# One program for the bias stage and attention, transposes ahead of scores, three more attention steps ahead of the MLP

## The chip, the core and the metric

The kernel runs on one core of a Trainium2 chip. The metric is the device time of one execution in microseconds. A core has TensorE (PE in the rows; its weight loads are PEld), VectorE (DVE), ScalarE (ACT), GpSimd (POOL) and SyncE (SP), which here only issues DMA transfers. Each engine runs its own list of instructions in order and waits on semaphores for the others.

## What is computed

Attention over 4 batches of 8 heads, 576 positions, 64 values a head, with a bias that a small network makes out of the distance of two positions; then two MLPs over the 2304 rows of 512 values.

```python
rel = (pos[:, None] - pos[None, :])
psi_rel, psi_i = log1p(abs(rel)), log1p(maximum(pos[:, None], 1.0))
x = (psi_rel / psi_i)[..., None]
bias = maximum(x @ w1 + b1, 0.0) @ w2              # 32 hidden values, 8 heads
scores = scale * q @ k.T + bias
attn = exp(scores - max) / (sum + 1e-9)
x = (attn @ v).transpose(0, 2, 1, 3).reshape(2304, 512)
h = x @ w_in;   x = (s * relu(h) ** 2 + b) @ w_out
h = x @ w2_in;  return (h - tanh(h)) @ w2_out      # d_ff is 2048 in both
```

## The kernel before

Every float32 operand of a large product is split in a rounded high part and a low part, so that a product is made of two or three matmuls. The program has three stretches.

**The bias stage.** 36 packs of 16 rows i. For each pack ScalarE and VectorE make two hidden tiles each (`hidden` and `maximum`), TensorE multiplies them by `w2_s` into one of four pairs of PSUM banks (`ps_f`, `ps_s`, `ps_t`, `ps_o`, in turn), ScalarE evicts the columns ahead of the diagonal and VectorE the mirrored ones behind it into `stage`, and SyncE stores the pack to the DRAM tensor `bias_flat`. A skewed view of it gives the bias rows of a head; `sp_bias` loads those of tile t into `bias_t`, which has one buffer for each tile. The hidden tiles have `HIDS` buffers, `stage` has four. This stage is a program block of its own, with a barrier of all engines at its end.

**Attention alone.** A head n is done in steps (n, t), t from 0 to 4, one for each tile of 128 query rows. A step carries three heads' work: scores of head n (`ps_s`, one pair of banks), VectorE's reduce L544, which adds the bias and takes the maximum, and ScalarE's exponential; transposes of head n-1's tile (L477, into `ps_t` and `ps_f` in turn while `alone`), ScalarE's rounding of it (`pth`, L490) and VectorE's low part (`ptl`, L556); and the value product of head n-1's previous tile (L442 and L444, `ps_o`). Step (n, 0) also ends head n-2: ScalarE copies the lower half (`o_tmp`), VectorE adds the halves into `x_raw`. The denominators are inverted on VectorE, transposed, stored in DRAM (`inv_rows`) and loaded again as a row for every partition (`inv_b`); in odd steps (n, 0) GpSimd scales two heads of `x_raw` by it (`pool_scale`). GpSimd also rounds k and makes the low parts of k, q and v of the heads to come; q and k have one raw buffer, so `load_qk` of head n+2 waits for the low parts of head n+1. The first 46 steps (`FIRST`) are done in this way.

**Mixed and MLP.** Then the MLP runs in units of 464 rows, 64 blocks of 12 matmuls each; after the blocks in `PLACES` of the first three units one attention step is put. `act_weights` and `pool_weights` split the weights three blocks ahead, `act_split` and `dve_split` split x.

```python
bias_t = tile("bias_t", [P, NT, S])
need(pe, min_done, n * NT + t)          # scores of a step wait for the reduce before
need(pe, pt_lo_done, v * NT + t - alone)
sp.wait_ge(min_done, n * NT + t + 1)    # SyncE, step (n, t), then bias rows of head n+1
```

Of the kernel before, what the change touches and what calls it, by code (L numbers as in the profile page):

```python
# [10 lines left out]
P = 128  # L11
# [7 lines left out]
HIDS = 3  # L19
VEC = 2  # L20
LATE = 2
RING = 4
# [4 lines left out]
def build(nc, qt, kt, vt, net, w2s, w2t, psi, lam, sb, w1, w2, w3, w4, out):  # L27
# [7 lines left out]
    HID = w2t.shape[0]  # L35
    G = P // HID
# [18 lines left out]
    FIRST = (H + 1) * NT + 1  # L55
# [5 lines left out]
    def step_at(u, k):  # L61

        if u >= B - 1 or k not in PLACES:
            return None
        return STEPS_AT[FIRST + u * H * NT + PLACES.index(k)]

# [12 lines left out]
    with ExitStack() as ctx:  # L79
# [26 lines left out]
        const_done = sem("const_done")  # L106
        hid_dve = sem("hid_dve")
        hid_act = sem("hid_act")
        no_const = sem("no_const")
# [94 lines left out]
        with ExitStack() as bctx:  # L204
            bb = lambda name, shape, dt=F32: bctx.enter_context(nc.sbuf_tensor(name, shape, dt))
            psi_t = bb("psi_t", [P, S])
            lam_c = bb("lam_c", [P, STEPS])
            inv_lam = bb("inv_lam", [P, STEPS])
            slope = bb("slope", [P, STEPS])
            net_c = bb("net_c", [P, 2])  # L210
            w1_c, b1_c = net_c[:, 0:1], net_c[:, 1:2]
            nb1_c = bb("nb1_c", [P, 1])
            w2_s = bb("w2_s", [P, G * H])
            w2_t = bb("w2_t", [HID, P])
            const = bb("const", [P, 1])
            hid = bb("hid", [P, HIDS, PACK, S])
            stage = bb("stage", [P, RES_BUFS, S + ROW])
            res = [ps_f, ps_s, ps_t, ps_o]

            def forward(pack):  # L220

                return S - pack * ROW

            def backward(pack):

                return pack * ROW + ROW - 1

            def reach(pack):

                n = max(forward(pack), backward(pack) + 1)  # L230
                return n + n % 2

            def chunks(pack):

                n = reach(pack)
                half = n // 2 + (n // 2) % 2
                parts = [(0, n)] if n <= BANK else [(0, half), (half, n)]
                return [(res[pack % RES_BUFS][:, c, 0:hi - lo], lo, hi) for c, (lo, hi) in enumerate(parts)]

            block = bctx.enter_context(nc.Block())  # L240

            def load_bias(sp, t):
                packs = min(PACKS, (t + 1) * P // ROW)
                for i in range(RES_BUFS):
                    sp.wait_ge(stage_stored[i], packs // RES_BUFS * DMA)
# [620 lines left out]
```

## Time and profile before

| | |
|---|---|
| three runs | 1181.2, 1181.64 and 1181.9 us, median 1181.64 |
| profiled execution | 1182.0 us, span of the trace 1180.2 us |
| TensorE busy | 1123.6 us, 95% of the span |
| ScalarE, VectorE, GpSimd busy | 720.2, 629.5 and 597.8 us |
| first bias hidden operation | 6.08 us |
| last mirrored bias row, start and length | 71.31 and 0.94 us |
| first attention reduce | 77.40 us |
| first MLP matmul | 180.49 us |
| DMA | 172.47 MB, most of it on SyncE's queue |

Times are counted from the start of the span. The engines' busy shares are means over stretches of very different kinds.

### The profile page before, as it was taken

The numbers are of one execution on the slowest core, as the hardware profiler recorded it, in microseconds if no ns is written. First come the engines' busy times: TensorE is split into PE (matmuls) and PEld (weight loads), VectorE is DVE, ScalarE is ACT, GpSimd is POOL, SyncE is SP. The second block draws the span as 40 slices with busy tenths as digits, with TensorE's granted clock in tenths as the row PEclk, the third lists the DMA queues.
The fourth block names the chain that finished last, engine by engine and source line by source line (L and its number), as shares of the span: only waits on it lengthen the run. The fifth ranks groups of instructions, "written<-read, shape, count | busy, mean of one in ns | idle before, by whom it ended". The sixth has DMA issues, their size and how long they took to land.

```text
span 1180.2 us, 17800 instructions
## 1 busy us (share of the span) xinstructions
PE 1123.6 (95%) x6306; PEld 995.0 (84%) x6306; DVE 629.5 (53%) x1090; ACT 720.2 (61%) x1362; POOL 597.8 (51%) x505
## 2 busy tenths in 40 slices
PE   4659878999999999999999999999999999999998
PEld 1138767999999999999999999999988888999998
DVE  5857775744675366447654754566344063260440
ACT  8957785755676477557665765676455264473552
POOL 1014545566465545655655555555455455555553
PEclk9879998999999999999999999999999999999999
DMA  3577773455445544554455454453233333433332
GB/s 127 209 249 200 217 211 93 151 172 178 139 155 159 175 152 142 163 157 141 162 167 171 138 160 156 149 162 125 81 115 107 107 101 105 131 109 124 97 111 75
DMA packets 69657, 172.47 MB, mean 146 GB/s; under 512 B 8704, under 2 KB 15680, under 8 KB 69568
## 3 DMA queue, kind: packets, MB, share of 16 engines
q1 hardware_dynamic: 69280, 171.24, 46.3%
q8 instruction: 51, 0.84, 0.3%
q14 instruction: 38, 0.31, 0.1%
q10 hardware_dynamic: 288, 0.07, 0.0%
HBM read 155.59 MB, written 15.69 MB: 145 GB/s over the span
## 4 chain that ended last, share of the span: by engine, by line
PE 85%; ACT 1%; issue 0%; DVE 0%; ACTq 0%
PE ps_f L652 23%; PE ps_f L654 23%; PE ps_f L653 23%; PE ps_t L477 6%; PE ps_o L442 3%; PE ps_o L444 3%; PE ps_s L464 3%; PE ps_s L465 3%; PE ps_s L458 0%; ACT p_t L499 0%; ACT pth L490 0%; DVE ptl L556 0%; ACT wh L602 0%; DVE xl L628 0%; DVE p_t L544 0%
## 5 line engine op out<-in xcount | busy, mean ns | idle before, releaser
L609 POOL TENSOR_TENSOR wl<-w_raw,wh 128x512 fp32r<-128x512 f32 x320 | 418.3, 1313 | 441.5 <-ACT wh L602 441.3
L652 PE MATMUL ps_f<-xh,wh 128*128 128x464 f32 (+1 forms) x640 | 239.4, 374 | 5.0 <-issue 5.0
L652 PE MATMUL ps_f<-gh,wh 128*128 128x464 f32 (+1 forms) x640 | 238.8, 373 | 0.0
L654 PE MATMUL ps_f<-xh,wl 128*128 128x464 f32 (+1 forms) x640 | 238.5, 373 | 0.0
L653 PE MATMUL ps_f<-xl,wh 128*128 128x464 f32 (+1 forms) x640 | 238.1, 372 | 0.0
L654 PE MATMUL ps_f<-gh,wl 128*128 128x464 f32 (+1 forms) x640 | 237.4, 371 | 0.0
L653 PE MATMUL ps_f<-gl,wh 128*128 128x464 f32 (+1 forms) x640 | 237.3, 371 | 0.0
L602 ACT ACTIVATE wh<-w_raw 128x512 fp32r<-128x512 f32 x320 | 198.0, 623 | 40.0 <-PE ps_f L654 39.8
L544 DVE CUSTOM_DVE_ANT_0 p_t<-ps_s,bias_t 128x576 f32<-128x576 f32 x160 | 120.0, 750 | 94.0 <-PE ps_s L465 93.3
L675 ACT ACTIVATE r_buf<-ps_f 128x464 f32<-128x464 f32 (+1 forms) x160 | 89.2, 557 | 115.0 <-PE ps_f L654 115.0
L490 ACT ACTIVATE pth<-ps_t 128x576 fp32r<-128x576 f32 (+1 forms) x140 | 91.0, 650 | 91.9 <-PE ps_t L477 89.7
L652 PEld LDWEIGHTS ps_f<-xh,wh 128*128 128x128 f32 x640 | 120.9, 189 | 17.8 <-issue 5.2
L499 ACT ACTIVATE p_t<-p_t,neg_max 128x576 f32<-128x576 f32 x160 | 123.0, 769 | 17.6 <-DVE neg_max L544 17.6
L654 PEld LDWEIGHTS ps_f<-xh,wl 128*128 128x128 f32 x640 | 120.8, 189 | 14.1
L654 PEld LDWEIGHTS ps_f<-gh,wl 128*128 128x128 f32 x640 | 120.1, 188 | 13.7
L653 PEld LDWEIGHTS ps_f<-xl,wh 128*128 128x128 f32 x640 | 120.8, 189 | 12.9
L653 PEld LDWEIGHTS ps_f<-gl,wh 128*128 128x128 f32 x640 | 120.1, 188 | 11.9
L652 PEld LDWEIGHTS ps_f<-gh,wh 128*128 128x128 f32 x640 | 120.1, 188 | 11.8
L556 DVE TENSOR_TENSOR ptl<-ps_t,pth 128x576 fp32r<-128x576 f32 (+1 forms) x140 | 105.4, 753 | 34.9 <-ACT pth L490 34.4
L464 PE MATMUL ps_s<-k2h,q 128*128 128x288 f32 x320 | 98.1, 321 | 11.7 <-DVE neg_max L544 6.7
L442 PE MATMUL ps_o<-pth,vhl 128*128 128x288 f32 x320 | 101.1, 331 | 5.9 <-DVE ptl L556 5.9
L703 DVE TENSOR_TENSOR gl<-g_buf,gh 128x464 fp32r<-128x464 f32 (+1 forms) x80 | 82.0, 1025 | 38.7 <-ACT gh L669 38.7
(74 smaller groups left out, 1536.6 us busy)
## 6 DMA issues: line engine op xcount, KB each, us to landing
w_raw<-in_w_in SPq DMA_DIRECT2D x80, 512.0 KB, 3.8
w_raw<-in_w_out SPq DMA_DIRECT2D x80, 512.0 KB, 3.7
bias_t<-bias_flat SPq DMA_DIRECT2D x128, 288.0 KB, 2.9
bias_flat<-stage SPq DMA_DIRECT2D x36, 295.5 KB, 2.1
q_raw<-in_qt SPq DMA_DIRECT2D x32, 288.0 KB, 3.9
k_raw<-in_kt SPq DMA_DIRECT2D x32, 288.0 KB, 4.5
v_raw<-in_vt SPq DMA_DIRECT2D x32, 160.0 KB, 4.1
bias_t<-bias_flat SPq DMA_DIRECT2D x32, 144.0 KB, 4.1
```

The source lines that it names most:

```text
L442: pe.matmul(ps_o[:, half, 0:HALF], vhl[:, n % 2, u, :], pth[:, slot(n, u), cols], start=(u == 0), stop=False)
L464: pe.matmul(acc, lhs, k2h[:, n % 2, cols], start=True, stop=False)
L490: act.activation(pth[0:R, slot(v, t), :], turn_bank(v, t, alone)[0:R, 0:S], ACT.Copy)\
L499: act.activation(p, p, ACT.Exp, scale=-1.0, bias=neg_max[:, t:t + 1], accum_out=den[:, n % 2, t:t + 1]).then_inc(exp_done, 1)
L544: dve.tensor_tensor_reduce(out=halves(p_t[:, n % 2, t, :]), in0=ps_s[:, :, 0:HALF], in1=halves(bias_t[:, t, :]), scale=-SCALE, scalar=3.0e ...
L556: dve.tensor_tensor(ptl[0:R, slot(v, t), :], turn_bank(v, t, alone)[0:R, 0:S], pth[0:R, slot(v, t), :].bitcast(F32), ALU.subtract).then_in ...
L602: act.activation(wh[:, b % RING, :, :], w_raw[:, b // 2 % RAW, b % 2, :, :], ACT.Copy)\
L609: pool.tensor_tensor(wl[:, b % RING, :, :], w_raw[:, b // 2 % RAW, b % 2, :, :], wh[:, b % RING, :, :].bitcast(F32), ALU.subtract).then_in ...
L652: pe.matmul(acc, hi, rhs_h[:, k0 + kk, 0:T], start=(first and kk == 0), stop=False)
L653: pe.matmul(acc, hi, rhs_l[:, k0 + kk, 0:T], start=False, stop=False)
L654: mm = pe.matmul(acc, lo, rhs_h[:, k0 + kk, 0:T], start=False, stop=(last and kk == 3))
L675: act.activation(r_buf[:, n % 2, 0:T], acc, (ACT.Relu, ACT.Tanh)[l]).then_inc(r_done, 1)
```

## The change

The bias stage moves into the one program block, as `sp_biases`, `act_biases`, `pool_biases`, `dve_biases` and `pe_biases`; its tiles lie in buffers that are free then (`carve`). The hidden layer is computed as max(psi w1 + lam b1, 0), and the division by lam is done in the evictions with a column `row_scale`. `HIDS` is 2. Head 0's scores alternate between `ps_s` and `ps_o`. In a step the transposes come ahead of the scores, the inverse is transposed at t = 3, the denominator is made in step 1. `load_qk(1)` is issued at pack 30, ahead of the last bias rows' load, and the first weight loads move to head 2. `FIRST` grows by 3. GpSimd splits the first three parts of x for the first unit, in heads 3, 5 and 7.

```diff
-HIDS = 3
+HIDS = 2
+EXTRA = 3
-    FIRST = (H + 1) * NT + 1
+    FIRST = (H + 1) * NT + 1 + EXTRA
...
-                        mm = act.activation(hid[:, pack % HIDS, at, 0:n], psi_t[:, 0:n], ACT.Relu,
-                                            scale=slope[:, step:step + 1], bias=b1_c)
+                    mm = act.activation(hid[:, pack % HIDS, at, 0:n], psi_w[:, 0:n], ACT.Relu,
+                                        bias=knee[:, step:step + 1])
...
-                            mm = act.activation(dst, acc[:, 0:hi - lo], ACT.Identity, scale=1.0 / SCALE,
-                                                bias=const[:, 0:1])
+                        mm = act.activation(dst, acc[:, 0:hi - lo], ACT.Copy,
+                                            scale=row_scale[:, pack:pack + 1])
...
-                        mm = dve.tensor_scalar(hid[:, pack % HIDS, at, 0:n], psi_t[:, 0:n],
-                                               slope[:, step:step + 1], nb1_c[:, 0:1], ALU.mult, ALU.max)
+                    mm = dve.tensor_scalar(hid[:, pack % HIDS, at, 0:n], psi_w[:, 0:n],
+                                           knee[:, step:step + 1], 0.0, ALU.add, ALU.max)
...
-                dve.wait_ge(net_loaded, 3 * DMA)
-                dve.wait_ge(psi_loaded, 2 * DMA)
-                dve.tensor_scalar(nb1_c[:], b1_c, -1.0, None, ALU.mult).then_inc(table_done, 1)
-                dve.reciprocal(inv_lam[:], lam_c[:]).then_inc(table_done, 1)
-                dve.wait_ge(table_done, 2)
-                dve.tensor_scalar(slope[:], inv_lam[:], w1_c, None, ALU.mult).then_inc(table_done, 1)
+            dve.tensor_scalar(psi_w, psi_t, w1_c, None, ALU.mult).then_inc(table_done, 1)
+            dve.tensor_scalar(knee, lam_c, b1_c, None, ALU.mult).then_inc(table_done, 1)
+            dve.reciprocal(row_inv, row_lam).then_inc(table_done, 1)
...
+                if pack == PACKS - 6:
+                    load_qk(sp, 1)
...
+        def pe_score(pe, n, t):
+            if t == 0:
+                pe.wait_ge(q_lo_done, n + 1)
+                pe.wait_ge(k_lo_done, n + 1)
+            if n == 0:
+                need(pe, min_done, t - 1)
+                pe.wait_ge(back_done, PACKS - 2 if t == 0 else PACKS)
+            else:
+                pe.wait_ge(min_done, n * NT + t)
...
+        def pe_turn_inv(pe, v):
+            pe.wait_ge(inv_done, v + 1)
+            need(pe, inv_row_done, v)
+            if scoring(v + 1):
+                pe.wait_ge(min_done, (v + 1) * NT + 3)
+            pe.transpose(ps_s[0:NT, 0, HALF:HALF + P], inv[:], ident[:]).then_inc(inv_turned, 1)
+
         def pe_step(pe, n, t, alone):
+            v = n - 1
+            if t and turning(n):
+                pe_turn(pe, v, t, alone)
+            if t == 3 and turning(n):
+                pe_turn_inv(pe, v)
...
+        def pool_split(pool, kt_):
+            T = UNITS[0]
+            pool.wait_ge(x_done, kt_ + 1)
+            pool.tensor_copy(xh[:, kt_, 0:T], x_raw[:, kt_, 0:T]).then_inc(x_hi_done, 1)
+            pool.wait_ge(x_hi_done, kt_ + 1)
+            pool.tensor_tensor(xl[:, kt_, 0:T], x_raw[:, kt_, 0:T], xh[:, kt_, 0:T].bitcast(F32),
+                               ALU.subtract).then_inc(x_lo_done, 1)
...
         @block.sync
         def _(sp):
-            load_qk(sp, 1)
-            for pair in range(RAW):
-                sp_weights(sp, pair)
+            sp_biases(sp)
             for n, t in STEPS_AT[:FIRST]:
+                if (n, t) == (0, 2):
+                    load_bias(sp, NT - 1)
                 sp_step(sp, n, t)
+                if n == 2 and t < RAW:
+                    sp_weights(sp, t)
...
             for n, t in STEPS_AT[:FIRST]:
                 pool_step(pool, n, t)
-            for b in range(AHEAD):
-                pool_weights(pool, b)
+                if t == 0 and n in (3, 5, 7):
+                    pool_split(pool, (n - 3) // 2)
+                if n == H and 0 <= t - NT + AHEAD:
+                    pool_weights(pool, t - NT + AHEAD)
...
-                if n == H and t == AHEAD:
-                    for kt_ in range(KD - 1):
-                        act_split(act, 0, kt_)
-            act_split(act, 0, KD - 1)
+                if (n, t) == (H + 1, 2):
+                    act_split(act, 0, KD - 1)
```

On SyncE, at the seam between the bias stage and attention, the program before has these rows (stores of packs, bias rows of head 0, then q and k of head 1, weights, bias rows of head 1):

```order
L262 DMA bias_flat<-stage 128x591 x8
L202 DMA bias_t<-bias_flat 128x576
L262 DMA bias_flat<-stage 128x591 x2
L202 DMA bias_t<-bias_flat 64x576
L204 UNCONDITIONAL_BRANCH
L729 UNCONDITIONAL_BRANCH
L171 DMA q_raw<-in_qt 128x576
L172 DMA k_raw<-in_kt 128x576
L594 DMA w_raw<-in_w_in 128x1024 x3
L202 DMA bias_t<-bias_flat 128x576 x4
```

The changed program has these at the same place; `w_raw` in the stores is where `stage` lies now:

```order
L287 DMA bias_flat<-w_raw 128x591 x5
L170 DMA q_raw<-in_qt 128x576
L171 DMA k_raw<-in_kt 128x576
L287 DMA bias_flat<-w_raw 128x591 x3
L201 DMA bias_t<-bias_flat 128x576
L287 DMA bias_flat<-w_raw 128x591 x2
L201 DMA bias_t<-bias_flat 128x576 x2
L201 DMA bias_t<-bias_flat 64x576
L201 DMA bias_t<-bias_flat 128x576 x2
```

The block's end is gone, q and k of head 1 stand five packs ahead of the end of the stores, the weights stand elsewhere, and the last bias rows of head 0 (64x576) stand behind two loads of head 1.

On GpSimd, in head 3 of attention, the program before has these rows (k's split, scaling of x, low part of q, v's split):

```order
L187 CAST k2h<-k_raw 128x576
L196 TENSOR_TENSOR k2l<-k_raw,k2h 128x576
L526 TENSOR_TENSOR x_raw<-x_raw,inv_b 128x576
L192 TENSOR_TENSOR q<-q_raw,q 128x576
L513 CAST vhl<-v_raw 128x5x64
```

The changed program has these:

```order
L186 CAST k2h<-k_raw 128x576
L195 TENSOR_TENSOR k2l<-k_raw,k2h 128x576
L536 TENSOR_TENSOR x_raw<-x_raw,inv_b 128x576
L542 CAST xh<-x_raw 128x464
L544 TENSOR_TENSOR xl<-x_raw,xh 128x464
L191 TENSOR_TENSOR q<-q_raw,q 128x576
L525 CAST vhl<-v_raw 128x5x64
```

Two operations on 464 columns of x stand between the scaling and the low part of q.

On VectorE, in step (2, 0) of attention and the start of (2, 1), the program before has these rows (reduce, its accumulator, sum of the halves, low part, denominator and inverse, reduce):

```order
L544 ISA p_t,neg_max<-ps_s,bias_t 128x576
L544 ISA neg_max 128x1
L552 TENSOR_TENSOR x_raw<-ps_o,o_tmp 64x576
L556 TENSOR_TENSOR ptl<-ps_f,pth 128x576
L564 TENSOR_SCALAR den_e<-den 128x5
L566 RECIPROCAL inv<-den_e 128x5
L544 ISA p_t,neg_max<-ps_s,bias_t 128x576
```

The changed program has these:

```order
L563 ISA p_t,neg_max<-ps_s,bias_t 128x576
L563 ISA neg_max 128x1
L571 TENSOR_TENSOR x_raw<-ps_o,o_tmp 64x576
L582 TENSOR_TENSOR ptl<-ps_f,pth 128x576
L563 ISA p_t,neg_max<-ps_s,bias_t 128x576
L563 ISA neg_max 128x1
L576 TENSOR_SCALAR den_e<-den 128x5
L578 RECIPROCAL inv<-den_e 128x5
L582 TENSOR_TENSOR ptl<-ps_t,pth 128x576
```

The denominator and its inverse moved from between the low part and the next reduce to behind that reduce.

## Rows read from the trace of the kernel before

**Rows 1.** Busy time by stretch: us, PE, PEld, DVE, ACT, POOL busy, PEclk, DMA, GB/s
```profile
45.00:54.00 9.00, 8.00 (x48) 1.27 (x48) 7.37 (x16) 8.88 (x17) 0.00 (x0) 0.54 0.56 218
57.00:69.00 12.00, 7.72 (x88) 2.24 (x80) 11.90 (x24) 12.00 (x23) 0.00 (x0) 1.00 0.59 213
...
180.00:190.00 10.00, 9.51 (x38) 8.49 (x39) 3.38 (x5) 3.24 (x6) 4.89 (x5) 0.68 0.19 54
190.00:300.00 110.00, 110.00 (x634) 101.01 (x633) 62.93 (x112) 70.42 (x135) 60.88 (x53) 1.00 0.52 160
```

**Rows 2.** Groups by line and form, 0 to 90 us: busy us, mean ns, idle before
```profile
L499 ACT ACTIVATE p_t<-p_t,neg_max 128x576 f32<-128x576 f32 x5 | 3.9, 777 | 11.5 <-DVE neg_max L544 11.5
L284 ACT ACTIVATE hid<-psi_t,net_c,slope 128x560 f32<-128x560 f32 x4 | 3.2, 860 | 0.0
...
L331 DVE RECIPROCAL inv_lam<-lam_c 128x144 f32<-128x144 f32 x1 | 1.0, 1043 | 0.0
```

**Rows 3.** Timeline of the first seam (start, us, engine); last row the page's DMA issues
```profile
71.31 0.94 DVE L352 TENSOR_SCALAR stage<-ps_o,const 128x287 f32<-128x287 f32 x2 [0.55 <-ACT stage L302]
...
74.50 0.51 SPq L202 DMA_DIRECT2D bias_t<-bias_flat  x1
...
77.40 0.76 DVE L544 CUSTOM_DVE_ANT_0 p_t<-ps_s,bias_t 128x576 f32<-128x576 f32 x1 [5.15 <-PE ps_s L465]
...
78.22 0.61 PE L464 MATMUL ps_s<-k2h,q 128*128 128x288 f32 x1 [0.96 <-DVE neg_max L544]
...
88.39 0.76 DVE L544 CUSTOM_DVE_ANT_0 p_t<-ps_s,bias_t 128x576 f32<-128x576 f32 x1 [1.48 <-PE ps_s L465]
...
bias_t<-bias_flat SPq DMA_DIRECT2D x32, 144.0 KB, 4.1
```

**Rows 4.** Timeline: head 3 from its first reduce, and head 8's first reduce
```profile
108.71 0.76 DVE L544 CUSTOM_DVE_ANT_0 p_t<-ps_s,bias_t 128x576 f32<-128x576 f32 x1
...
108.84 0.40 PE L442 MATMUL ps_o<-pth,vhl 128*128 128x288 f32 x1 [0.17 <-DVE ptl L556]
...
110.35 0.75 DVE L552 TENSOR_TENSOR x_raw<-ps_o,o_tmp 64x576 f32<-64x576 f32 x1 [0.88 <-ACT o_tmp L485]
...
111.13 0.76 DVE L556 TENSOR_TENSOR ptl<-ps_t,pth 128x576 fp32r<-128x576 f32 x1
...
111.81 0.16 DVE L564 TENSOR_SCALAR den_e<-den 128x5 f32<-128x5 f32 x1
...
112.12 0.76 DVE L544 CUSTOM_DVE_ANT_0 p_t<-ps_s,bias_t 128x576 f32<-128x576 f32 x1
...
161.22 0.75 DVE L544 CUSTOM_DVE_ANT_0 p_t<-ps_s,bias_t 128x576 f32<-128x576 f32 x1
```

**Rows 5.** Timeline of SyncE's queue and GpSimd in head 3
```profile
107.93 0.43 SPq L172 DMA_DIRECT2D k_raw<-in_kt  x1
...
112.83 0.67 POOL L187 CAST k2h<-k_raw 128x576 fp32r<-128x576 f32 x1 [5.75 <-DMA k_raw<-in_kt]
113.57 1.44 POOL L196 TENSOR_TENSOR k2l<-k_raw,k2h 128x576 fp32r<-128x576 f32 x1
...
117.72 0.46 POOL L513 CAST vhl<-v_raw 128x320 fp32r<-128x320 f32 x1
```

**Rows 6.** Timeline of the second seam, from head 9's first scores
```profile
173.58 0.37 PE L464 MATMUL ps_s<-k2h,q 128*128 128x288 f32 x1 [2.20 <-DVE neg_max L544]
...
174.39 0.76 DVE L544 CUSTOM_DVE_ANT_0 p_t<-ps_s,bias_t 128x576 f32<-128x576 f32 x1 [0.29 <-PE ps_s L465]
...
179.20 0.59 ACT L622 ACTIVATE xh<-x_raw 128x464 fp32r<-128x464 f32 x1 [2.14 <-POOL x_raw L526]
...
180.49 0.72 PE L652 MATMUL ps_f<-xh,wh 128*128 128x464 f32 x1 [5.00 <-issue]
```

**Rows 7.** Timeline of TensorE in the mixed stage, one attention step
```profile
241.82 0.29 PE L464 MATMUL ps_s<-k2h,q 128*128 128x288 f32 x1
...
243.42 0.38 PE L652 MATMUL ps_f<-gh,wh 128*128 128x464 f32 x1
```

More of the change, by code:

```diff
@@ new lines, in reach, with chunks, load_bias @@
+        def reach(pack):
+            n = max(forward(pack), backward(pack) + 1)
+            return n + n % 2
+        def chunks(pack):
+            n = reach(pack)
+            half = n // 2 + (n // 2) % 2
+            parts = [(0, n)] if n <= BANK else [(0, half), (half, n)]
+            return [(res[pack % RES_BUFS][:, c, 0:hi - lo], lo, hi) for c, (lo, hi) in enumerate(parts)]
+        def load_bias(sp, t):
+            packs = min(PACKS, (t + 1) * P // ROW)
+            for i in range(RES_BUFS):
+                sp.wait_ge(stage_stored[i], packs // RES_BUFS * DMA)
+            if t == NT - 1:
+                sp.wait_ge(bias_clear, 1)
+            sp_bias(sp, 0, t)
@@ new lines, in sp_biases @@
+        def sp_biases(sp):
+            sp.dma_start(psi_t, psi).then_inc(psi_loaded, DMA)
+            sp.dma_start(w2_s, w2s).then_inc(net_loaded, DMA)
+            sp.dma_start(row_lam, lam_rows).then_inc(net_loaded, DMA)
+            sp.dma_start(sb_c[:], sb.to_broadcast((P, 2))).then_inc(sb_loaded, DMA)
+            load_qk(sp, 0)
+            load_v(sp, 0)
+            for pack in range(PACKS):
+                back, ahead = backward(pack), forward(pack)
+                sp.wait_ge(back_done, pack + 1)
+                rows = bias_rows[pack * P:(pack + 1) * P, S - back:S + ahead]
+                sp.dma_start(rows, stage[:, pack % RES_BUFS, 0:back + ahead])\
+                    .then_inc(stage_stored[pack % RES_BUFS], DMA)
+                t, late = divmod(pack - LATE + 1, P // ROW)
+                if t and not late:
+                    load_bias(sp, t - 1)
+                if pack == PACKS - 6:
+                    load_qk(sp, 1)
@@ new lines, in pe_biases @@
+        def pe_biases(pe):
+            pe.wait_ge(net_loaded, 3 * DMA)
+            for pack in range(PACKS):
+                need(pe, back_done, pack - RES_BUFS + 1)
+                pe.wait_ge(hid_dve, pack + 1)
+                pe.wait_ge(hid_act, pack + 1)
+                for acc, lo, hi in chunks(pack):
+                    for at in range(PACK):
+                        mm = pe.matmul(acc[at * G * H:(at + 1) * G * H, :], w2_s,
+                                       hid[:, pack % HIDS, at, lo:hi], start=True, stop=True)
+                mm.then_inc(hid_used, 1)
```

354 lines of the change are left out of this document (150 added, 204 removed).

## The prediction

> **What bounds the kernel now.** I read the busy time by stretch first. From 190 to 300 us TensorE (PE) is busy for 110.00 of 110 us at full clock [rows 1]; in that mixed stage, where MLP blocks and attention steps alternate, only less TensorE work helps. Two matmul starts one step apart (first score, first MLP matmul behind it) give the price of a step there: 243.42 - 241.82 = 1.60 us [rows 7]. So what can be won lies ahead of the MLP, which starts at 180.49 [rows 6]. There I read four things. In the bias stage ScalarE (ACT) is busy 12.00 of 12 us from 57 to 69, VectorE (DVE) 11.90, TensorE 7.72; but from 45 to 54, at a mean granted clock of 0.54, which is mostly the lower level of 1.2 GHz, TensorE is busy for 8.00 of 9 [rows 1]. At the first seam the last bias row leaves VectorE at 71.31 + 0.94 = 72.25 and its first attention reduce starts at 77.40: 5.15 us of nothing [rows 3]. In the attention-only stretch no engine is full; the first reduces of heads 3 and 8 stand at 108.71 and 161.22 [rows 4], so a head takes 52.51 / 5 = 10.50 us. Head 8, which also carries the splits of x, takes 174.39 - 161.22 = 13.17, and at the second seam TensorE idles 5.00 us ahead of the first MLP matmul [rows 6].
>
> **Opening.** ACT's first hidden operation waited for VectorE's reciprocal of 144 columns, 1.04 us [rows 2], and a multiply. Now it waits for a multiply of 576 columns and a small one; the reciprocal that is left has 36 columns and lies beside ACT's work. I take -0.5 us (0 to -1).
>
> **Bias stage.** Each pack keeps two hidden operations on ACT, but these now have one per-partition operand (a bias column) where they had two (scale and bias columns). The trace has both kinds: 128x560 with two takes 860 ns, the exponential with one takes 777 ns for 128x576, 16 columns more [rows 2]; the difference is 83 ns plus what 16 columns cost, about 95. I take 90 ns for each of 72 operations if ACT ends the cycle. Of 36 packs I leave out eight that run at the low clock, where TensorE nearly fills the time, so 28 x 2 x 0.09 = 5.0; in the last eight VectorE is as full as ACT and loses less, for which I give back 0.7. Result -4.3 (0 to -6.5). The buffer of hidden rows shrinks from three to two, so VectorE's hidden(p) waits for TensorE's pack p-2; its program puts the mirrored rows of pack p-3 before it, and those need ACT's eviction, hence TensorE's pack, p-3. The wait is then for a matmul group of about a us that started a cycle earlier. I cost it at nothing; if VectorE were pushed by 0.3 us in each of the eight full packs, 2.4 us would be lost. The Trainium skill, page "ScalarE: Activation LUTs", section "What ACT_TABLE_LOAD costs", states about 93 ns for each pointer operand whatever the function; by it the full sum would be 6.7 us. No run here has yet changed the operand alone.
>
> **First seam.** The barrier between the two programs goes. Scores of head 0 start when pack 33's bank is free, and alternate between two banks. VectorE can start its first reduce at about 72.3 instead of 77.40. With one bank a cycle was reduce to score 0.82 us (77.40 to 78.22) [rows 3] and score to reduce; at full clock the latter is 174.39 - 173.58 = 0.81 [rows 6]. With two banks four reduces are over by about 77. Then the fifth waits for the last bias rows. That load was issued at 74.50; it now stands behind head 1's first two loads, so about 75.0, and such a load lands in 4.1 us at the median [rows 3]: 79.1. Then 0.8 to the score and 1.1 to head 1's first reduce (half way between clock levels): 81.0 against 88.39. I take -7.5 (-6 if the load is slow, -9 if it lands in 3). Head 1's own q and k are loaded at pack 30 and split long before, and the 1.5 MB of weights are no longer in the queue here. Head 1 itself: -0.2.
>
> **Each head.** The gap from reduce 0 to reduce 1 is 112.12 - 108.71 = 3.41 us. In it stand a value product (108.84), the sum of the halves (110.35), the low part (111.13) and the denominator (111.81), which takes 112.12 - 111.81 = 0.31 [rows 4]. The denominator moves behind reduce 1, -0.3. With transposes ahead of scores the low part of the previous tile is ready earlier and its value product with it, -0.25. What follows is not all gain: step 1 now needs value product, transposes and scores in a row on TensorE before reduce 2, and at step 3 the copy of the reciprocals, which waits for the scores, stands ahead of the reduce. I get +0.1 and +0.3 there. The last two gaps can fall to the loop of 0.82 + 0.81 = 1.63, -0.25 together. Sum -0.4 a head; six heads (2 to 7) -2.4 (0 to -5).
>
> **GpSimd.** In head 3 the load of k is issued at 107.93 and its split starts at 112.83; split of k, scaling of x and low part of q end at 117.72, 4.89 us later and 9.01 after the head's first reduce [rows 4, 5]. The next head's scores could come 10.50 - 0.81 = 9.69 after it, a slack of 0.7 us. Now q and k are issued ahead of the load of the reciprocals, some 1.1 us earlier. But in heads 3, 5 and 7 GpSimd also splits 464 columns of x: a cast, 0.67 x 464/576 = 0.54, a subtraction, 1.16 by the same share of the 1.44 of rows 5, and a wait, 1.75 in all. The two gaps between the load's reduce and the next head are 0.3 shorter. So the low part of q ends at 9.01 - 1.1 + 0.3 + 1.75 = 9.96, and the next scores could start at 10.1 - 0.8 = 9.3: 0.7 late. The late q also holds the next load on SyncE, since q and k have one raw buffer, so heads 5 and 7 are 1.1 late each. The three weight loads, 512 KB each, spread over head 2, add 0.7 to head 4's k. Sum +3.6 (0 to +8). Without this queue the splits would cost nothing: GpSimd was idle for 5.75 us ahead of each head's first split [rows 5].
>
> **Head 8 and second seam.** Three of the four splits are gone from ACT and VectorE; head 8 then takes a usual 10.1 and 0.4 for the weight casts: -2.7. From head 9's first reduce to the MLP it was 180.49 - 174.39 = 6.1 us, ended by the scaling of x on GpSimd, its split at 179.20, and VectorE's part [rows 6]. Now three more steps stand here: reduces at +2.85, +4.8, then ACT's last split at about +7, VectorE's low part to +8.4, the reduce behind it and its low part, +10.0. So +3.9 (+2 to +6). In return three steps leave the mixed stage: 3 x 1.60 = -4.8. From 180 to 190 the clock was 0.68 [rows 1], that is 6.4 us at the lower level, 3.2 lost. TensorE's idle time ahead of the MLP falls from 5.0 to about 3; idle of 2.20 ahead of 173.58 [rows 6] did not lower the clock. I take -2.4 (0 to -3.2). In the mixed stage itself the new order costs nothing: TensorE is never short of MLP work.
>
> **Sum.** -0.5 - 4.3 - 7.5 - 0.2 - 2.4 + 3.6 - 2.7 + 3.9 - 4.8 - 2.4 = -17.3. The profiled execution took 1182.0 (span 1180.2, 1.8 around it), so 1164.7; the median shown is 0.4 lower, so 1164.3.
>
> **The rivals.**
> A, the forecast: 0.50, own range 1160 to 1169.
> B, the bias stage gains nothing, because the difference of rows 2 belongs to the function and not the operand, or because TensorE's low clock or the short buffer ends the cycle: 1164.3 + 4.3 = 1168.6. For it: the 8.00 of 9. Against: ACT is full in most packs. 0.15.
> C, GpSimd becomes the bound. If each of three heads is late by 3.5 instead of about 1: +7.5, 1171.8. For it: 0.7 us of slack and one raw buffer. Against: the earlier issue. 0.12.
> D, the loop falls to 1.63 in four gaps and GpSimd hides its splits: 3.6 + 2.4, 1158.3. For it: no engine is full. 0.15.
> E, slower than before: TensorE's clock stays at 1.2 GHz in the attention-only stretch. A step's 1.60 us of work would be 3.2, a head 16.0 against 10.1, 5.9 more; three heads at the low clock use up the 17.3, and eight would give 1164.3 + 47 = 1211. For it: head 0 ran at the low level (a score of 0.61 us at 78.22 [rows 3] against 0.37 at 173.58 [rows 6]) between thin groups of scores, and the extra waits of the three odd heads make new gaps. Against: the stretch held the high level with such gaps in it. The Trainium skill, "TensorE: Matmul & The Clock Gate", section "A second HAM failure mode: psum-queue depth-cycling", has a kernel whose short idle times between groups made the clock go back and forth; by that rule E is real. The trace of before bears it out only in the bias stage. 0.04.
> F, it does little: the waits of the seams only change their name, for instance because the last bias rows or q come later than I read; within 0.2%: 0.04.
>
> **How the numbers follow.** About 0.2%, 2.4 us, is what a measurement of this kernel can tell from no change. A, B, C and D are faster: 0.92. F is 0.04 the same, E 0.04 slower. The range reaches from D's time less 2 to C's plus 1, 1156 to 1173; it leaves out E, F and half of the outer tails of C and D, near 2 in 10.
>
> **What the profile would show.** The hidden operations at 128x576 near 0.79 us, or B. VectorE's last mirrored row near 67.5, its first reduce within 0.3 of it, head 1's first reduce near 76, head 9's near 162, the first MLP matmul near 171 with little at the low clock behind it. In heads 3, 5 and 7 the scores of the next head wait for GpSimd's low part of q; if heads 4, 6 and 8 start without such a wait, the GpSimd term is wrong. TensorE's busy time from the MLP's start on should be 4.8 us less. The prediction is wrong above all if that last stretch is not shorter, or if the odd heads take 12 us and more.

## The result, and the profile of the changed kernel

The changed kernel takes 1170.96 us in the median of 4 runs (1168.46 to 1173.01), before it 1181.42: a ratio of 0.991 (95% interval 0.9885 to 0.9936). Run once more beside the experiments it took 1168.86 (1167.88 to 1171.26), ratio 0.9893 (0.9879 to 0.9906). So it is 10 to 13 us faster; forecast were 17.3. The profiled execution took 1172.88 against 1182.0, so 9.1 less.

The page shows that TensorE is still busy nearly all the time, and in its last row, in tenths for each fortieth of the span, that its clock is nearly always full:

```profile
PE 1119.2 (96%) x6304; PEld 993.9 (85%) x6304; DVE 620.2 (53%) x1087; ACT 713.6 (61%) x1358; POOL 603.8 (52%) x511
...
PEclk9989999999999999999999999999999999999999
```

The bias stage, as groups by form (busy us, mean ns of one), and then the first seam in VectorE's timeline (start, length in us):

```profile
L305 ACT ACTIVATE x_raw<-y 128x576 f32<-128x576 f32 x4 | 2.9, 787 | 2.6 <-DVE y L348 2.6
L305 ACT ACTIVATE x_raw<-y 128x560 f32<-128x560 f32 x4 | 2.8, 771 | 0.0
...
L358 DVE TENSOR_SCALAR x_raw<-y 128x576 f32<-128x576 f32 x4 | 1.9, 515 | 0.0
```

```profile
64.20 0.94 DVE L369 TENSOR_SCALAR w_raw<-ps_o,y 128x287 f32<-128x287 f32 x2 [0.56 <-ACT w_raw L322]
65.06 0.75 DVE L563 CUSTOM_DVE_ANT_0 p_t<-ps_s,bias_t 128x576 f32<-128x576 f32 x1
...
72.89 0.76 DVE L563 CUSTOM_DVE_ANT_0 p_t<-ps_s,bias_t 128x576 f32<-128x576 f32 x1 [4.44 <-DMA bias_t<-bias_flat]
...
75.14 0.76 DVE L563 CUSTOM_DVE_ANT_0 p_t<-ps_s,bias_t 128x576 f32<-128x576 f32 x1 [1.49 <-PE ps_s L455]
```

ScalarE's hidden operation of 560 columns takes 771 ns against 860 [rows 2], and the last mirrored row ends at 65.14 against 72.25 [rows 3]. The fifth reduce of head 0 waits for the last bias rows; head 1 starts 13.25 us earlier than before. The chain of work that ended last shows (start, length in us) what it waits for, the last store and the load behind it:

```profile
65.17 4.76 DMA bias_flat<-w_raw
70.07 2.69 DMA bias_t<-bias_flat
```

Head 1 starts a little earlier than the sum gave (76.1). The loss comes behind it. From head 1's first reduce to head 9's were 86.00 us before [rows 3, 6]; I expected 84.3, and it is 167.36 - 75.14 = 92.22. The lengths of the heads, from first reduce to first reduce, are 11.31, 11.22, 13.56, 11.32, 11.26, 10.00, 12.10 and 11.45 us. Head 6 has what a head costs when nothing comes in its way. The timeline of VectorE and GpSimd in head 2 and of GpSimd in head 3 shows the two things that do; the last row is head 4's first reduce:

```profile
89.09 0.75 DVE L563 CUSTOM_DVE_ANT_0 p_t<-ps_s,bias_t 128x576 f32<-128x576 f32 x1
...
89.76 1.41 DVE L576 TENSOR_SCALAR den_e<-den 128x5 f32<-128x5 f32 x1
91.21 0.19 DVE L578 RECIPROCAL inv<-den_e 128x5 f32<-128x5 f32 x1
91.31 0.72 DVE L582 TENSOR_TENSOR ptl<-ps_t,pth 128x576 fp32r<-128x576 f32 x1
91.95 0.75 DVE L563 CUSTOM_DVE_ANT_0 p_t<-ps_s,bias_t 128x576 f32<-128x576 f32 x1
...
89.72 1.43 POOL L195 TENSOR_TENSOR k2l<-k_raw,k2h 128x576 fp32r<-128x576 f32 x1
...
103.04 0.66 POOL L186 CAST k2h<-k_raw 128x576 fp32r<-128x576 f32 x1 [8.78 <-DMA k_raw<-in_kt]
103.79 1.41 POOL L195 TENSOR_TENSOR k2l<-k_raw,k2h 128x576 fp32r<-128x576 f32 x1
105.42 1.42 POOL L536 TENSOR_TENSOR x_raw<-x_raw,inv_b 128x576 f32<-128x576 f32 x1 [0.22 <-issue]
106.91 0.57 POOL L542 CAST xh<-x_raw 128x464 fp32r<-128x464 f32 x1
107.56 1.17 POOL L544 TENSOR_TENSOR xl<-x_raw,xh 128x464 fp32r<-128x464 f32 x1
108.68 1.39 POOL L191 TENSOR_TENSOR q<-q_raw,q 128x576 fp32r<-128x576 f32 x1
...
111.23 0.76 DVE L563 CUSTOM_DVE_ANT_0 p_t<-ps_s,bias_t 128x576 f32<-128x576 f32 x1 [2.72 <-PE ps_s L455]
```

VectorE's addition for five columns takes 1.41 us where it took 0.16 [rows 4], and it ends with GpSimd's subtraction for k, at 91.17 and 91.15. So it is in heads 1, 2, 5 and 9 (1.04 to 1.41 us), in part in head 4 (0.66). I call this a collision. The profile of before already had one, in head 9:

```profile
177.13 0.71 DVE L564 TENSOR_SCALAR den_e<-den 128x5 f32<-128x5 f32 x1
...
176.41 1.41 POOL L196 TENSOR_TENSOR k2l<-k_raw,k2h 128x576 fp32r<-128x576 f32 x1
```

There too both end together, at 177.84 and 177.82. Head 4 starts after a wait of 2.72 us for scores that need q's low part, head 8 after 2.30. The late load also holds head 3 in a second way, through ScalarE, which rounds q ahead of the next `pth`:

```profile
103.01 0.78 ACT L181 ACTIVATE q<-q_raw,lower 128x576 fp32r<-128x576 f32 x1 [0.94 <-DMA k_raw<-in_kt]
...
104.36 0.76 DVE L582 TENSOR_TENSOR ptl<-ps_t,pth 128x576 fp32r<-128x576 f32 x1 [1.12 <-ACT pth L500]
```

This is why head 3's gap from reduce 2 to 3 is 2.76 us where head 6 has 1.95.

The windows (PE, PEld, DVE, ACT, POOL busy, PEclk, DMA share, GB/s) show a third loss, TensorE's clock, in four places:

```profile
73.00:81.00 8.00, 6.91 (x32) 6.68 (x33) 4.91 (x11) 4.78 (x10) 2.43 (x3) 0.58 0.71 216
...
110.00:120.00 10.00, 9.45 (x58) 8.69 (x58) 6.87 (x16) 6.09 (x13) 6.13 (x8) 0.83 0.66 194
...
150.00:160.00 10.00, 7.95 (x46) 7.13 (x45) 6.15 (x15) 5.80 (x14) 6.16 (x7) 0.83 0.61 188
...
178.00:188.00 10.00, 10.00 (x47) 8.88 (x47) 4.25 (x7) 4.71 (x9) 2.60 (x2) 0.83 0.43 143
```

Each stands behind an idle time of TensorE, of 5.49, 2.56, 1.85 and 2.37 us. The first MLP matmul starts at 177.78 (180.49 before), and from there to the end it is 993.3 us, before 999.7.

### The profile page after: what moved, and what is told of

It reads as the page before. It is cut to its first block, busy times and chain, and to the rows that moved or that the text cites. A ratio compares the mean times of both kernels' runs of the same rounds, so it can differ in the third digit from the quotient of the medians.

```text
span 1171.1 us, 17786 instructions
## 1 busy us (share of the span) xinstructions
PE 1119.2 (96%) x6304; PEld 993.9 (85%) x6304; DVE 620.2 (53%) x1087; ACT 713.6 (61%) x1358; POOL 603.8 (52%) x511
## 4 chain that ended last, share of the span: by engine, by line
PE 88%; ACT 5%; DMA 2%; DVE 2%; issue 1%; POOL 1%; SPq 0%; ACTq 0%; DVEq 0%; POOLq 0%
PE ps_f L677 23%; PE ps_f L675 23%; PE ps_f L676 23%; PE ps_t L465 6%; PE ps_o L435 3%; PE ps_s L454 3%; PE ps_o L437 3%; PE ps_s L455 3%; ACT x_raw L305 2%; ACT w_raw L322 1%; DMA inv_rows<-inv_row 1%; DVE p_t L563 1%; DVE ptl L582 1%; PE ps_f L465 1%; DMA inv_b<-inv_rows 0%
## 5 line engine op out<-in xcount | busy, mean ns | idle before, releaser
L454 PE MATMUL ps_s<-k2h,q 128*128 128x288 f32 x316 | 101.0, 334 | 11.5 <-DVE neg_max L563 7.1
L582 DVE TENSOR_TENSOR ptl<-ps_t,pth 128x576 fp32r<-128x576 f32 (+1 forms) x138 | 102.6, 743 | 9.2 <-ACT pth L500 8.6
L435 PE MATMUL ps_o<-pth,vhl 128*128 128x288 f32 x320 | 93.8, 309 | 9.0 <-DVE ptl L582 8.9
L723 DVE SCALAR_TENSOR_TENSOR gl<-g_buf,sb_c,gh 128x464 fp32r<-128x464 f32 (+1 forms) x80 | 78.5, 982 | 44.3 <-ACT gh L688 44.3
```

The costliest lines, as they stand in the source:

```text
L435: pe.matmul(ps_o[:, half, 0:HALF], vhl[:, n % 2, u, :], pth[:, slot(n, u), cols], start=(u == 0), stop=False)
L454: pe.matmul(acc, lhs, k2h[:, n % 2, cols], start=True, stop=False)
L582: dve.tensor_tensor(ptl[0:R, slot(v, t), :], turn_bank(v, t, alone)[0:R, 0:S], pth[0:R, slot(v, t), :].bitcast(F32), ALU.subtract).then_in ...
```

## The experiments

Every time is the median of 4 to 10 executions, with the lowest and the highest behind it. The kernel before, measured beside each of the three groups of runs, took 1182.07, 1181.98 and 1182.08 us, so the groups can be compared. "Start of the MLP" is the start of the first MLP matmul in the profile, and "rest" the span less that.

**The changed kernel again.**

> The changed kernel once more, unedited, as the base of the edits that run beside it. Its four times lay at 1168.5 to 1169.0 and at 1172.9 to 1173.0. All theories expect 1168 to 1174 us here. If its times again lie in two groups 4 us apart, single times of the edits can be read to 4 us only, and medians and the parts of the trace have to decide.

1168.86 us (1167.88 to 1171.26). In its profile the addition collides in heads 2 and 5 (1.35 and 1.43) and not in head 1 (0.17): whether it does depends on when k lands. In head 1 GpSimd's subtraction starts 3.38 us behind the first reduce in the first profile and 2.41 in this one, where it is nearly over when the addition starts. The four executions lay up to 4.5 us apart the first time and 3.4 now, and the two medians of this one kernel are 2.1 apart, so a difference of medians of 2 us or less shows nothing without the profile. That the collisions make this spread is not shown, since both profiled executions are among the longer ones of their four.

**The addition back in step 0.**

```diff
-            if t == 1 and turning(n):
...
             if between:
                 between()
+            if t == 0 and turning(n):
...
```

The block under the condition, with the addition and the reciprocal, moves along unchanged, from ahead of the low part to behind it.

> Denominator and reciprocal on VectorE go back from step 1 to the end of step 0; all else as in the changed kernel. Theory 1 (collision): in heads 1, 2, 5 and 9 the 128x5 addition takes 1.04 to 1.41 us because GpSimd's subtraction for k runs then and VectorE's operation ends only with it; the place of the addition is what costs. Then the addition takes 0.16 us again in every head, the gap from reduce 1 to reduce 2 in heads 1, 2 and 5 falls from 2.63-2.86 to about 2.05, the gap from reduce 0 to 1 grows by 0.3, and the time falls by 2 to 4 us. Rival: the addition merely fills time in which VectorE waits for TensorE's transposes and scores; then the gap stays near 2.7 and the time changes by less than 1 us, or grows by 0.3 a head (2 us).

1174.24 us (1172.05 to 1174.38), ratio 0.9933 (0.9919 to 0.9947): 5.4 slower than the changed kernel, against my theory. In attention alone it did what theory 1 said, 0.16 to 0.18 us in heads 2, 3, 5, 6, 7 and 8 and the gap from reduce 1 to 2 at 1.65 to 1.73, but head 1 (1.38) and head 4 (0.56) collided in the new place. In head 4 it was not the subtraction but the cast ahead of it: the addition ends at 112.71, GpSimd's cast of k (112.02, 0.67 us long) at 112.69. The first MLP matmul stands at 174.46. The rest is 995.8 us, though, 2.5 more, and the waits of TensorE from 190 on, which are none in the changed kernel, are

```profile
PE ps_f L675 <- DVE g_buf L735: 1.9, 3, 0.6
```

By this profile step 1 is the better place in the mixed stage, where in step 0 VectorE is late for the MLP's `g_buf`. The profiled executions of the two kernels are only 0.8 apart, though (1172.05, the fastest of its kernel, and 1171.26, the slowest), so most of the 5.4 between the medians stays unexplained.

**GpSimd's splits of x behind q's low part.**

```diff
-                if t == 0 and n in (3, 5, 7):
+                if t == 2 and n in (3, 5, 7):
                     pool_split(pool, (n - 3) // 2)
```

> GpSimd's split of x in heads 3, 5 and 7 moves from step 0 (ahead of the low part of q) to step 2 (behind it). Theory 2 (GpSimd queue): head 4 and head 8 start late because q's low part stands behind k's split, the scaling and this split of 1.75 us. Then the waits ahead of the first reduces of heads 4 and 8 (2.72 and 2.30 us) fall to about 1.0 and 0.5, heads 3 and 7 take 11.8 and 10.4 instead of 13.56 and 12.1, and the time falls by 3 to 4 us. Rival: what is late is the load of k and the reload of the reciprocals, and the queue closes up behind them whatever stands in it; then the waits fall by less than 0.5 and the time by less than 1 us. A third way: the first low clock stretches behind these waits (0.83 in 110 to 120 and 150 to 160) vanish as well, which would add up to 1.5 us of gain each.

1165.94 us (1165.02 to 1166.48), 2.9 faster, a little less than the 3 to 4 expected. Head 7 takes 10.39 and head 8 starts without a wait (0.28); the clock of 150 to 160 is 1.00. Head 3 still takes 12.22: GpSimd is free, but k and the reciprocals come late:

```profile
102.70 0.67 POOL L186 CAST k2h<-k_raw 128x576 fp32r<-128x576 f32 x1 [8.69 <-DMA k_raw<-in_kt]
...
105.84 1.42 POOL L536 TENSOR_TENSOR x_raw<-x_raw,inv_b 128x576 f32<-128x576 f32 x1 [0.98 <-issue]
107.23 1.40 POOL L191 TENSOR_TENSOR q<-q_raw,q 128x576 fp32r<-128x576 f32 x1
```

Of the 2.2 us over a free head, 0.8 is the third gap (2.80), which ScalarE's late rounding of q makes as before.

**The first weights' loads in head 5.**

```diff
-                if n == 2 and t < RAW:
+                if n == 5 and t < RAW:
                     sp_weights(sp, t)
```

> The three first weight loads (512 KB each) move from head 2 to head 5. Theory 2b: they stand ahead of head 4's k on the queue, which lands 6.8 us after its issue and holds GpSimd idle for 8.8 us in head 3. Then k lands 1.5 to 2.5 us earlier, head 3 takes 11.3 to 12 instead of 13.56, the clock of 110 to 120 stays at 1.00, and the time falls by 1.5 to 3 us; head 6 or 7 may give back 0.5. Rival: the reload of the reciprocals (stored at 96.9, landed at 105.2) sets GpSimd's time in head 3 and not k; then head 3 keeps 13 us or more and the time changes by less than 0.7 us.

1167.21 us (1165.46 to 1168.04), 1.7 faster, which the medians alone would not settle. Head 3 takes 11.69, with k's cast here:

```profile
98.70 0.67 POOL L186 CAST k2h<-k_raw 128x576 fp32r<-128x576 f32 x1 [6.03 <-DMA k_raw<-in_kt]
```

That is 3.74 us behind the head's first reduce (94.96), where it was 103.04 - 97.67 = 5.37, and head 3's third gap is 1.95. So the weight loads delay what stands behind them on the queue, as theory 2b says. Whether k or the reciprocals set GpSimd's time is not separated: the store of the reciprocals took 5.54 us before this edit and 3.90 behind it, and in both profiles the reload landed (105.20 and 100.87) as the subtraction for k ended. Head 6 pays with 11.20.

**Both moves.**

> Both moves that gained alone: GpSimd's splits of x at step 2 of heads 3, 5 and 7 (alone 1165.9 against 1168.9 for the changed kernel) and the weight loads in head 5 (alone 1167.2). If the queue theory holds and the two lateness terms are separate, head 3 takes about 10.3 instead of 13.56 to 14.33, head 7 about 10.4, the first MLP matmul stands near 168.5 and the time is 1163 to 1164. Rival: each move only takes away the same wait, so together they give no more than the better one, 1165.5 to 1166.5.

1164.54 us (1162.7 to 1165.91). The waits ahead of the heads are gone (0.28 to 0.36), so the two terms are separate. Two things keep the time above the expected 1163 to 1164: the addition now collides in heads 2, 3 and 4 (1.16, 1.17, 1.09), and the weight loads delay head 6 (12.15), where ScalarE waits 2.06 us for q and k. The first MLP matmul stands at 170.69, expected was 168.5.

**Both moves, no addition.** The 1e-9 is left out of the denominators.

```diff
-                dve.tensor_scalar(den_e[:], den[:, v % 2, :], 1e-9, None, ALU.add).then_inc(den_done, 1)
-                dve.wait_ge(den_done, v + 1)
-                dve.reciprocal(inv[:], den_e[:]).then_inc(inv_done, 1)
+                dve.reciprocal(inv[:], den[:, v % 2, :]).then_inc(inv_done, 1)
```

> The two moves, and the addition of 1e-9 to the denominators is left out: VectorE only inverts them (128x5 reciprocal, 0.19 us so far always just behind the addition). Theory 1a: it is the addition as an operation that collides, because it takes both of VectorE's ways into SBUF, and a reciprocal doesn't. Then no head shows a gap from reduce 1 to 2 above 2.1 us, whatever GpSimd does, the third gap is 1.96 everywhere, and the time falls by about 1.2 us for each collision that the kernel with two moves still has (2 to 3 of them): 2 to 4 us below it. Theory 1b: any operation there collides with GpSimd's subtraction; then the reciprocal takes up to 1.4 us in the same heads and the time stays within 0.7 us.

**Both moves, the addition in another form.**

```diff
-                ... 1e-9, None, ALU.add).then_inc(den_done, 1)
+                ... 1e-9, 0.0, ALU.add, ALU.add, accum_out=den_sum[:]).then_inc(den_done, 1)
```

> The two moves, with the addition kept, but in the form that also writes the sum of its results into a column (a second output that nothing reads). Theory 1a with its mechanism: the form of the operation decides whether it waits for GpSimd. Then the addition takes 0.3 us or less in every head (a little more than 0.16 for the sum), gaps 1 to 2 stay at 2.2 us or less, and the time is that of the kernel without the addition plus 0 to 1 us. Rival: the form changes nothing, and the addition takes up to 1.4 us in the heads in which GpSimd subtracts at that time.

1163.85 us (1162.56 to 1166.82) and 1165.12 (1164.07 to 1166.81), against 1164.54 with the plain addition. The 2 to 4 us expected did not come: both medians are the same as that within their spread, and the verdict rests on the profiles. In both no head has a gap from reduce 1 to 2 above 2.22 us, and from head 2 on it is 2.04 to 2.06. Without the addition, GpSimd's subtraction lay over the reciprocal in heads 1 and 9 alone (0.18 and 0.19 us). With the sum it lay over the addition in heads 2, 3 and 4, and the addition took 0.15 us in each. So it does in head 2 of the next kernel, which has this form:

```profile
88.42 0.15 DVE L577 TENSOR_SCALAR_CACHE_REDUCE den_e<-den 128x5 f32<-128x5 f32 x1
88.50 0.08 DVE L577 DVE_READ_ACCUMULATOR den_e<-den 128x1 f32 x1
88.62 0.19 DVE L580 RECIPROCAL inv<-den_e 128x5 f32<-128x5 f32 x1
...
88.20 1.43 POOL L195 TENSOR_TENSOR k2l<-k_raw,k2h 128x576 fp32r<-128x576 f32 x1
```

Theory 1a is shown: it is the form of the operation that waits for GpSimd. The Trainium skill, page "SBUF — State Buffer", section "Who interferes with whom", says that an operation like the plain `tensor_scalar` can take a pair of ports that VectorE shares with GpSimd, that the one that comes second waits for the whole instruction of the other, and that the form with an accumulated output does not take it. The rows agree, 1.41 against 0.15 us, and both engines' operations end together in the first case. From head 1 to head 9 the form with the sum needs 83.2 us against 86.3 of the kernel with both moves, but the median does not follow: 1165.12 against 1164.54. Its profile has the MLP start at 168.71, 2.0 earlier, and a rest of 993.6 against 991.7, since the clock falls again ahead of the MLP; in head 6 (11.59), behind the weight loads, 1.6 us are lost.

**A second per-partition operand on ScalarE.**

```diff
 mm = act.activation(hid[:, pack % HIDS, at, 0:n], psi_w[:, 0:n], ACT.Relu,
+                    scale=one[:, 0:1],
                     bias=knee[:, step:step + 1])
```

> The changed kernel with a second per-partition operand in ScalarE's hidden operation: a scale column that holds 1.0. The result is the same. Theory 3: a per-partition operand costs about 90 ns on ScalarE whatever the function, which is what shortened the bias stage: 128x576 goes from 787 back to about 878 ns, the last mirrored row ends 4 to 6.5 us later (65.1 or 64.2 to about 69 to 70), and the time grows by 4 to 6. Rival: the stage became shorter because VectorE's hidden operation lost an operand too (575 to 515 ns) or because of the evictions; then ScalarE's operand costs less than 2 us of the stage.

1178.83 us (1177.33 to 1181.83), 8 to 10 slower than the two medians of the changed kernel, where 4 to 6 were expected. The operand costs 90 ns, and the last mirrored row ends at 71.23, 6.1 later than in the profile of the changed kernel and 7.1 later than in its second one (64.17):

```profile
L306 ACT ACTIVATE x_raw<-y,one 128x576 f32<-128x576 f32 x4 | 3.3, 877 | 2.6 <-DVE y L350 2.6
```

Theory 3 is shown for the bias stage. Against the first profile of the changed kernel the profiled execution is 8.9 us longer: beside these 6.1 us, 1.0 arises in the heads (93.22 against 92.22; heads 3, 5 and 7 take 14.24, 12.78 and 12.16), 2.6 from the MLP's start on (995.9 against 993.3, at the same granted clock), and the seams give 0.8 back. I take it that the heads meet the loads at other times, which no run shows by itself; the 2.6 are left open.

**One weight load to a head**, with GpSimd's splits at step 2 and the addition with the sum: the base of the last three.

```diff
-                if n == 2 and t < RAW:
-                    sp_weights(sp, t)
+                if t == 4 and n in (3, 4, 5):
+                    sp_weights(sp, n - 3)
```

> The base of this group: the accumulating form of the addition, GpSimd's splits at step 2, and the three weight loads one each at step 4 of heads 3, 4 and 5 instead of three in a row in head 5. In the kernel with three loads in head 5 all heads took 10.0 to 10.1 us but head 6, 11.6, and head 8, 10.7. Theory (the queue of loads): three loads of 512 KB in a row delay what comes behind them, one at a time does not. Then head 6 takes 10.0 to 10.3 and the time is 1162.5 to 1164. Rival: each single load now delays its own head by 0.5; then there is no gain, 1164 to 1166.

1162.83 us (1161.85 to 1164.68), ratio 0.9843 (0.983 to 0.9856). Head 6 takes 10.04 where it took 11.59 with three loads in a row, head 3 10.47; from head 1 to head 9 it is 82.05 us.

**Matmuls that nothing reads, in TensorE's idle times.**

```diff
+                if (n, t) == (1, 0):
+                    pe_fill(pe, 1, 28)
                 pe_step(pe, n, t, True)
+            pe_fill(pe, H + 1, 12)
             pe.wait_ge(pt_lo_done, H * NT + EXTRA + 1)
```

`pe_fill(pe, n, count)` waits for k of head n and multiplies a part of `k2h` by another into `ps_t`, 128x288, `count` times.

> The base of this group with matmuls that nothing reads: 28 of 128x288 (0.135 us each at the high clock) ahead of head 1's first scores, where TensorE is idle for 5.5 to 6.1 us, and 12 ahead of the MLP, where it is idle for 2.4 to 3.1. Theory 4 (clock): it is these idle times that bring the granted clock down to 0.50 just behind them. Then 73 to 81 and the first ten us of the MLP stay at 1.00, head 1's gap from reduce 0 to 1 falls from 3.10 to about 2.65, the span behind the first MLP matmul is 991.7 or less in the profile, and the time falls by 1.5 to 3 us against the base, with less spread among the runs. Rival: the clock falls for another reason (the power of the bias stage's end, or a fixed pattern in time), or the matmuls come in the way of the first score; then the time is the same or up to 1 us more.

1160.90 us (1159.8 to 1161.91), ratio 0.9822 (0.9808 to 0.9835): the fastest version, 1.9 below the base, at the lower end of what was expected, and 8 to 10 below the changed kernel, with the least spread of the group. The ranges of the two only touch, and the profiled executions differ by 2.05. Its timeline of TensorE and its windows:

```profile
67.45 3.84 PE L479 MATMUL ps_t<-k2h 128*128 128x288 f32 x28
73.55 0.37 PE L455 MATMUL ps_s<-k2h,q 128*128 128x288 f32 x1 [2.25 <-DVE neg_max L569]
```

```profile
73.00:81.00 8.00, 6.95 (x51) 6.23 (x52) 5.71 (x16) 6.28 (x13) 4.08 (x5) 1.00 0.78 226
...
165.00:175.00 10.00, 9.28 (x49) 8.39 (x50) 4.91 (x8) 5.57 (x11) 2.98 (x3) 1.00 0.50 156
```

The same windows of the base have 0.63 and 0.83. Head 1's first gap falls from 3.10 to 2.16 us, more than the 2.65 expected, and the rest is 992.3 us (base 993.9, expected 991.7 or less). For the first idle time theory 4 holds: in all twelve profiles of the changed kernel and its edits without these matmuls the clock from 73 to 81 was 0.57 to 0.76, and with them it is 1.00. Ahead of the MLP it is likely but not shown, since three kernels without filling matmuls (both moves, no addition, scores ahead) also had 1.00 there, behind 2.85, 2.39 and 2.37 us.

**Scores ahead of the transposes.**

```diff
-            if t and turning(n):
-                pe_turn(pe, v, t, alone)
             if t == 3 and turning(n):
                 pe_turn_inv(pe, v)
             if scoring(n):
                 pe_score(pe, n, t)
+            if t and turning(n):
+                pe_turn(pe, v, t, alone)
```

> The base of this group, but in a step the scores stand ahead of the transposes on TensorE again. The prediction gave the new order 0.25 us for the value product that is ready earlier and 0.25 for the last two gaps, less 0.4 for steps 1 and 3, so it is worth little by itself: heads take 10.0 to 10.3, the time changes by -1 to +2 us. Rival: the order is what brought a head from 10.5 to 10.0 us; then heads take 10.4 or more and the time grows by 3 to 4 us.

1166.47 us (1164.1 to 1168.25), 3.6 slower than the base. So the rival's time came, but its heads of 10.4 and more only in part. Heads 2 to 7 take 10.30 and 10.40, by gaps of 3.01, 1.65, 2.12, 1.63 and 1.90 where the base has 2.64, 2.05, 1.95, 1.63 and 1.73. So the order is worth 0.3 us a head. From head 1 to 9 that is 83.39 - 82.05 = 1.3; the profiled executions are 2.2 apart, and what of the 3.6 is more than that is left open.

**No extra steps.**

```diff
-EXTRA = 3
+EXTRA = 0
...
-                if (n, t) == (H + 1, 2):
+                if (n, t) == (H + 1, 0):
                     act_split(act, 0, KD - 1)
```

VectorE's `dve_split` moves in the same way.

> The base of this group with no extra steps ahead of the MLP (the last split of x at step 0 of head 9 on ScalarE and VectorE). The prediction: three steps cost 3.9 us ahead of the MLP and give back 4.8 in the mixed stage and up to 2.4 of clock, net -0.9 to -3.3. Then the first MLP matmul stands 3.5 to 4.5 us earlier than in the base, the rest of the span is 4.8 to 7 us longer, and the time is 1 to 3 us more. Rival: the steps are worth nothing, since a step ahead of the MLP costs 1.45 us of time for 1.6 saved; then the time is within 1 us of the base.

1163.94 us (1161.87 to 1166.47), 1.1 slower than the base, with ranges that overlap, so the medians don't tell it from no change. The MLP starts at 160.95, 5.3 earlier, but stops again for ScalarE's and VectorE's last split:

```profile
166.63 0.76 PE L677 MATMUL ps_f<-xh,wh 128*128 128x464 f32 x1 [3.53 <-DVE xl L653]
```

The clock is 0.71 from 161 to 171, and the rest is 1003.8 against 993.9. Without the idle 3.5 and the low clock (about 3.5 us lost against 1.7) that is 4.6 for three steps. From head 9's first reduce on, the base needs 9.79 + 993.9 us and this kernel 2.88 + 1003.8, so in the profiles the extra steps are worth 3.0.

## Why the prediction was right and where it was wrong

The time, 1171.0, lies in the range (1156 to 1173), 6.7 above the forecast and outside the forecast's own 1160 to 1169; run again, the kernel took 1168.86. That the range held owes something to luck, as shown under the rivals. In the profiled execution the gain was 9.1 where 17.3 stood, and by my own steps the 8.2 come from these places.

**Bias stage and opening: larger.** Forecast -4.8, measured 65.14 - 72.25 = -7.1. The opening is right: ScalarE's first hidden operation starts at 5.52 instead of 6.08. That leaves -6.5 for the stage. The mechanism was right, and its price too: 90 ns for an operand (771 against 860, and 877 with the operand given back). The step that failed is "of 36 packs I leave out eight" and the 0.7 given back. All 72 operations count, 72 x 0.09 = 6.5; giving the operand back alone cost 6.1 to 7.1. The reason given, that TensorE fills the low-clock packs, was wrong: ScalarE was busy for 8.88 of the 9.00 us there too [rows 1]. In the changed kernel the same stretch, 45 to 54 us, ran at a clock of 0.97 where it was 0.54, which I hadn't foreseen and for which I have no cause. VectorE's hidden operation also lost one operand, 575 to 515 ns for 576 columns, which I hadn't priced. Buffers of two hidden tiles were never tried against three; with the price of the operand making up the whole gain, there is no room for the loss of 2.4 that I feared.

**First seam: smaller, together nearly right.** From the last mirrored row to head 1 it is 75.14 - 65.14 = 10.0, before 16.14, so -6.1 for -7.5. The last load did land fast (2.69), but the store ahead of it took 4.76. Head 1 starts at 75.14; the sum gave 76.1.

**The heads: the terms that failed.** Forecast for head 1's to head 9's first reduce 84.3, measured 92.22. By the prediction's own sign, odd heads of 12 us and more, this part of it was wrong: heads 3 and 7 took 13.56 and 12.10. A head without a disturbance takes 10.0, forecast 10.1; the order gives 0.3 of the difference to before. Two prices were wrong.
- "The denominator moves behind reduce 1, -0.3": I asked what it costs there and not who else works then. GpSimd's subtraction for k lies over it. The gap from reduce 1 to 2 rises from 2.05 to 2.79-2.86 and the next from 1.96 to about 2.38, 1.2 us for heads 2 and 5, 0.9 for head 1 (against the same head in the second profile) and 0.5 for head 4: 3.8 in all. That is the missing term.
- "GpSimd, +3.6": head 3 is 3.5 over a free head and head 7 2.1, while head 5 isn't late by this at all. The place was right, the sizes were not: k comes 1.6 us later behind the weight loads (0.7 forecast), and the low clock behind the wait adds to the next head: the first gaps of heads 4 and 8 are 3.49 and 3.38, against 2.56 to 2.64 without the wait. Together that is 3.5 + 2.1 + 2 x 0.8 = 7.2, so 3.6 over the forecast. I had also reckoned with one path alone, over GpSimd to the next head's scores; 0.8 of head 3's 3.5 came over ScalarE's rounding of q.

With 3.8 and 3.6 these two make up 7.4 of the 7.9 us.

**Second seam: right.** Head 9's first reduce to the MLP took 177.78 - 167.36 = 10.4, forecast 10.0. The splits leave ScalarE and VectorE, and head 8 has 10.6 in the kernels without the wait (10.1 and 0.4 forecast).

**Three steps and the clock: right.** From the MLP's start on 993.3 against 999.7, -6.4 for -7.2. Some 3.4 us stay at the low level (0.83 over ten us), 1.7 lost where 3.2 were. So the clock gives -1.5 for -2.4, and the steps -4.9 for -4.8; TensorE's busy time from there on fell by the same 6.4 (996.8 to 990.3). What the extra steps bring as a whole is less sure, 1.1 us in medians whose ranges overlap and 3.0 in the profiles, where -0.9 to -3.3 were forecast.

**The rivals.** B fell with the operand's 90 ns. C had the right mechanism at too high a price: 3.6 + 7.5 = 11.1 us for the lateness where 7.2 were measured. Its time, 1171.8, is nearly the measured one, but by luck: the collision, which no rival had, made up the rest. D's premise didn't come: of the five gaps of a free head only one is 1.63 (the others are 2.64, 2.05, 1.95 and 1.73). E is there in small: no long fall of the clock, but four short ones, each behind a wait. With the first and the last idle time filled, 1.9 us came back.

## What to carry to other kernels

A small VectorE operation is not small if GpSimd works at that time: before moving it, look at what GpSimd's row shows in the new place, and take a form of the operation that doesn't wait for it. In the profiles this made heads 2, 3 and 4 together 2.8 us shorter; the medians, which also hold what changed elsewhere, did not show it. When one engine's queue carries work that the next stage needs, put what nobody waits for behind it. Put one large load, not three, between small ones with a deadline. When TensorE must wait, the price is the wait and often a low clock behind it; matmuls that nothing reads were worth 1.9 us here.

## What the runs showed of the hardware

- A VectorE addition of 128x5 elements took up to 1.41 us beside a GpSimd subtraction, 0.56 beside the end of a GpSimd cast, and 0.15 beside a subtraction in the form that also writes a sum. A reciprocal of the same tile took 0.19 beside it.
- TensorE's clock fell behind single waits of 5.49, 2.56, 2.37 and 1.85 us, but stayed at 1.00 behind one of 2.85 (the kernel with both moves, ahead of the MLP) and, at the same place, behind 2.39 (no addition) and 2.37 (scores ahead of the transposes): the length of the last wait alone doesn't decide. 3.84 us of unread matmuls in an idle time of about 6 kept it at 1.00, though 2.25 us of idle were left.
- Store and load of the last bias rows have lengths of 4.76 and 2.69 us where 144 KB loads took 4.1 at the median [rows 3]. Two profiles of one program have the load of k 1.0 us apart in head 1, with a collision in one (1.04 us) and none in the other (0.17); its executions differ by up to 4.5 us, and what makes them differ is open.
